# Gathering the first block of tokens before the last two expert tiles are stored

## What is computed

```python
def _moe_ref(x, w_gate, w_noise, noise, w1, w2):
    ...
    for e in range(E):                      # 8 experts
        for k in range(2):                  # a token's two best
            mask = top2[:, k] == e
            h = np.maximum(x[mask] @ w1[e], 0.0)
            out[mask] += top2_w[mask, k, None] * (h @ w2[e])
    return out

def _moe2_ref(x, w_in, w_out):              # x: 1152 x 512, w_in: 512 x 2048
    h = x @ w_in
    g = h * np.cos(h)
    return g @ w_out
```

## Time and profile before

| | before |
|---|---|
| median of 3 runs | 867.7 us (865.75 to 868.94) |
| the profiled execution | 867.97 us, its span 866.2 us |
| PE busy | 845.9 us, 98% of the span |
| DVE, ACT, POOL busy | 493.7, 421.9, 401.3 us |
| granted TensorE clock | 0.998 of full, mean |
| chain that ended last | PE 88%, DVE 5%, ACT 2%, POOL 2% |

### The profile page before, as it was taken

The page is one execution under the profiler, slowest core; times in us unless marked ns, Lnnn a source line. Parts: engine busy times, 40 slices in busy tenths (PEclk is TensorE's granted clock), DMA queues, the critical chain, the costliest instruction groups (busy, mean ns, idle before and its releaser), DMA issues.

```text
span 866.2 us, 15441 instructions
## 1 busy us (share of the span) xinstructions
PE 845.9 (98%) x4894; PEld 751.0 (87%) x4895; DVE 493.7 (57%) x983; ACT 421.9 (49%) x775; POOL 401.3 (46%) x293
## 2 busy tenths in 40 slices
PE   7999999999999989999999999999988999999998
PEld 6899999999999887888888888888877889999897
DVE  6788778887778886323232323232234776575664
ACT  3777777777777763211121112111134565565544
POOL 8554445546787006567959956859022030000000
PEclk9999999999999999999999999999999999999999
DMA  5212111152251017986536636445225020100101
GB/s 133 63 42 79 46 41 41 41 159 63 89 165 49 1 56 236 339 296 222 171 111 219 201 133 194 133 147 181 73 84 183 1 73 1 37 1 0 38 1 37
DMA packets 51377, 90.50 MB, mean 104 GB/s; under 512 B 9360, under 2 KB 18576, under 8 KB 50832
## 3 DMA queue, kind: packets, MB, share of 16 engines
q1 hardware_dynamic: 40688, 66.47, 23.2%
q10 hardware_dynamic: 7296, 12.59, 4.5%
q0 software_dynamic: 3360, 11.01, 4.2%
HBM read 73.00 MB, written 17.06 MB: 104 GB/s over the span
## 4 chain that ended last, share of the span: by engine, by line
PE 88%; DVE 5%; ACT 2%; POOL 2%; issue 1%; DMA 1%; another core or an unknown queue 0%; DVEq 0%; POOLq 0%; ACTq 0%
PE ps L1583 10%; PE ps L1585 10%; PE ps L1584 10%; PE ps L1405 5%; PE ps L1435 4%; PE ps L1451 4%; PE ps L1453 4%; PE ps L1452 4%; PE ps L1436 4%; PE ps L1684 3%; PE ps L1683 3%; PE ps L1682 3%; PE ps L1667 3%; PE ps L1669 3%; PE ps L1668 3%; PE ps L1622 2%
## 5 line engine op out<-in xcount | busy, mean ns | idle before, releaser
L623 POOL TENSOR_TENSOR W<-stage,W 128x2048 fp32r<-128x2048 f32 x32 | 147.2, 4600 | 2.6
L999 DVE TENSOR_REDUCE mx<-ps 128x1 f32<-128x384 f32 x225 | 119.6, 551 | 18.2 <-PE ps L1405 18.2
L1011 DVE TENSOR_TENSOR pl__77<-ps,ph 128x576 fp32r<-128x576 f32 x144 | 108.0, 750 | 33.5 <-ACT ps L775 33.5
L770 ACT ACTIVATE ph<-ps 128x576 fp32r<-128x576 f32 x144 | 93.9, 652 | 53.4 <-PE ps L1436 52.4
L775 ACT ACTIVATE ps<-ps 128x576 f32<-128x576 f32 x144 | 93.5, 649 | 0.0
L844 ACT CAST hh<-ps 128x512 fp32r<-128x512 f32 x50 | 26.9, 590 | 129.4 <-PE ps L1622 125.9
L1451 PE MATMUL ps<-ph,vs 128*65 128x288 f32 x288 | 86.0, 299 | 0.4 <-ACT ot L729 0.4
L1435 PE MATMUL ps<-qat,kt 128*128 128x288 f32 x288 | 83.7, 306 | 1.3 <-ACT qbt L722 0.6
L1453 PE MATMUL ps<-ph,vs 128*65 128x288 f32 x288 | 84.8, 294 | 0.0
L1452 PE MATMUL ps<-pl__77,vs 128*65 128x288 f32 x288 | 84.6, 294 | 0.0
L1583 PE MATMUL ps<-W,hh 128*128 (+1 forms) x200 | 80.0, 400 | 1.8 <-DVE hl L1269 1.8
(11 more groups left out here) (210 smaller groups left out, 1966.6 us busy)
## 6 DMA issues: line engine op xcount, KB each, us to landing
stage<-in_moe_w_dram SPq DMA_DIRECT2D x32, 1024.0 KB
y_slots<-ys ACTq DMA_DIRECT2D x25, 256.0 KB
x_slots<-ring SPq DMA_DIRECT2D x22, 256.0 KB
xs<-x_slots ACTq DMA_DIRECT2D x22, 256.0 KB
kn<-in_k_dram SPq DMA_DIRECT2D x16, 288.0 KB, 3.3
vn<-in_v_dram SPq DMA_DIRECT2D x16, 288.0 KB, 2.9
stage<-in_moe_w_in_dram SPq DMA_DIRECT2D x4, 1024.0 KB
stage<-in_moe_w_out_dram SPq DMA_DIRECT2D x4, 1024.0 KB
```

What stands on the lines that cost most here:

```text
L623: pl.tensor_tensor(W[:, slot, 1, part], stage[:, j % 2, :], W[:, slot, 0, part].bitcast(F32), ALU.subtract).then_inc(w_ready, 1)
L999: ve.tensor_reduce(mx3[:, i:i + 1], ps[:, bank_of(hh, ("m", i)), 0:PIECE], AX_X, ALU.max).then_inc(m_ev, 1)
L1011: ve.tensor_tensor(pl_[:, j % 3, :].rearrange("p (a n) -> p a n", a=2), ps[:, 2 * s_par(hh, j):2 * s_par(hh, j) + 2, 0:HQ], ph[:, j % 3, : ...
```

## The change

The first block of tokens (tiles 0 to 2) is gathered when the first 23 tiles are stored (`LATE = SLOTS_T - 2`). A position at or above 23 x 128 is replaced by 0, and its gate by 0 (`pos_on`, `gate_on`), so a token whose row is in tile 23 or 24 gets nothing for it from the gather. That part comes from two matrices `late_sel` of 128 slots x 384 tokens with a token's gate where its slot is, and 0 elsewhere. DVE makes them from the route table, which SP broadcasts to all partitions as `rtb`. PE multiplies `ys` of tile 23 and of tile 24 with them straight into four PSUM banks (0, 1, 4 and 6, one for each 128 of the 512 numbers), which gives the turned tokens, and adds the turned gathered tokens into the same banks by matmuls with the identity. ACT and DVE then split these banks into `fh` and `fl` at once. The matmuls on old data are gone. SP's handling of the route table moves from behind expert 7's weights to ahead of expert 3's. Blocks 1 and 2 are gathered and turned as before, once all 25 tiles are stored.

```diff
-WARM_Y = 38
-WARM_F = 8
+LATE = SLOTS_T - 2
+X2_BANKS = (0, 1, 4, 6)
...
@@ SP
-            with sp.Fori(3, E) as e:
-                stage_set(WPIECES * e, expert_pieces(e))
             sp.wait_ge(route_done, 1)
...
             sp.dma_start(rt2[:, :, :], route.rearrange("(i p) f -> p i f", p=P)).then_inc(rt_loaded, 16)
+            sp.dma_start(rtb[:, :, :].rearrange("p t f -> p (t f)"),
+                         route[0:BLK, :].rearrange("t f -> (t f)").partition_broadcast(P)).then_inc(rtb_loaded, 16)
+            with sp.Fori(3, E) as e:
+                stage_set(WPIECES * e, expert_pieces(e))
@@ POOL
-            pool.wait_ge(y_stored, 16 * SLOTS_T)
+            pool.wait_ge(y_stored, 16 * LATE)
             for i in range(TT):
+                if i == BLK_T:
+                    pool.wait_ge(y_stored, 16 * SLOTS_T)
@@ ACT
             def tile_steps(t, first=False, left=3, more=None, stored=0):
+                if left == 0:
+                    scale_first(0)
+                    scale_first(1)
                 move_h(t)
                 if not first:
                     store_y(t - 1)
+                if left == 0:
+                    scale_first(2)
...
-            for step in TILE_STEPS:
-                for i, part in step:
-                    (scale_first, high_f)[part](i)
+            for c in range(DC):
+                act.wait_ge(bt_done, c + 1)
+                sc.copy(fh[0][:, c, :], ps[:, X2_BANKS[c], 0:BLK]).then_inc(bh_ev, 1)
@@ DVE
+            def late_tiles():
...
+                dve.wait_ge(rtb_loaded, 16)
+                for k in range(2):
+                    for n in range(2):
+                        last = ve.scalar_tensor_tensor(late_n[:, n, :], rtb[:, :, n], late_slot[:, k:k + 1], rtb[:, :, 2 + n],
+                                                       ALU.is_equal, ALU.mult)
+                    then(last)
+                    then(ve.tensor_tensor(late_sel[:, k, :], late_n[:, 0, :], late_n[:, 1, :], ALU.add))
...
             def tile_steps(t, left=3, first=False):
+                if left == 1:
+                    late_tiles()
                 low_h(t)
+                if left == 0:
+                    add_second(1)
+                    add_second(2)
+                    low_out(0)
+                    low_out(1)
...
+                if left == 1:
+                    add_second(0)
...
+            for c in range(DC):
+                dve.wait_ge(bh_ev, c + 1)
+                ve.tensor_tensor(fl[0][:, c, :], ps[:, X2_BANKS[c], 0:BLK], fh[0][:, c, :].bitcast(F32), ALU.subtract
+                                 ).then_inc(bl_ev, 1)
...
+                if g == 0:
+                    dve.wait_ge(y_stored, 16 * SLOTS_T)
@@ PE
+            def late_rows(k):
+                pe.wait_ge(y_ev, LATE + k + 1)
+                for c in range(DC):
+                    last = pe.matmul(ps[:, X2_BANKS[c], 0:BLK], ys[:, c * P:(c + 1) * P], late_sel[:, k, :],
+                                     start=(k == 0), stop=(k == 1))
+                    if k == 1:
+                        last.then_inc(bt_done, 1)
+            def add_tokens(i):
+                pe.wait_ge(x2_done, i + 1)
+                for c in range(DC):
+                    last = pe.matmul(ps[:, X2_BANKS[c], i * P:(i + 1) * P], yg[:, i, 0, c * P:(c + 1) * P], ident[:, :],
+                                     start=False, stop=False)
+                last.then_inc(ft_done, 1)
             def tile_steps(t, left=3):
                 turn_h(t)
...
+                if left == 0:
+                    late_rows(0)
+                    add_tokens(0)
+                    add_tokens(1)
                 expert_out(t)
+                if left == 0:
+                    add_tokens(2)
+                    late_rows(1)
...
-            for i in range(WARM_Y):
-                pe.matmul(ps[:, 3, :], hh[:, i % FC, :], W[:, 0, 0, 0:BANK], start=True, stop=True)
-            for m in range(BLK_T):
-                turn_tokens(m)
-                for i in range(WARM_F):
-                    pe.matmul(ps[:, 3, :], hh[:, i % FC, :], W[:, 0, 0, 0:BANK], start=True, stop=True)
```

More of the change, by code:

```diff
@@ L388, in build @@
         assert at <= REGION + REGION_BYTES
+        assert at <= XD + 10240
+        rtb, at = place("rtb", XD + 10240, [P, BLK, 4])
+        late_sel, at = place("late_sel", at, [P, 2, BLK])
+        assert at <= REGION + REGION_BYTES
+        late_n, at = place("late_n", REGION + BLK_T * 2 * DM * 4, [P, 2, BLK])
         yg, at = place("yg", REGION, [P, BLK_T, 2, DM])
@@ L861, in high_half, with scale_first @@
                 sc.copy(W[:, 1, 0, at:at + HALF], stage[:, j, part * HALF:(part + 1) * HALF]).then_inc(oh_done, 1)
+            def scale_first(i):
+                act.wait_ge(gather_in[i % BLK_T], 16 * (i // BLK_T + 1))
+                first = yg[:, i % BLK_T, 0, :]
+                gate = gate_on[:, i, 0:1] if i < BLK_T else rt2[:, i, 2:3]
+                sc.activation(first, first, ACT.Copy, scale=gate).then_inc(xa_done, 1)
             def tile_steps(t, first=False, left=3, more=None, stored=0):
+                if left == 0:
+                    scale_first(0)
+                    scale_first(1)
                 move_h(t)
@@ L891, in _ @@
             store_y(SLOTS_T - 1)
[L894 to L898, removed]
             def high_f(i):
@@ L1276, in move_y, with add_second @@
                 ve.tensor_copy(ys[:, :], ps[:, 5, :]).then_inc(y_ev, 1)
+            def add_second(i):
+                dve.wait_ge(xa_done, i + 1)
+                dve.wait_ge(second_in[i % BLK_T], 16 * (i // BLK_T + 1))
+                first = yg[:, i % BLK_T, 0, :]
+                gate = gate_on[:, i, 1:2] if i < BLK_T else rt2[:, i, 3:4]
+                ve.scalar_tensor_tensor(first, yg[:, i % BLK_T, 1, :], gate, first, ALU.mult, ALU.add).then_inc(x2_done, 1)
+            def late_tiles():
+                dve.wait_ge(rt_loaded, 16)
+                then(ve.scalar_tensor_tensor(pos_on[:, :, :], rt2[:, 0:BLK_T, 0:2], float(LATE * P), rt2[:, 0:BLK_T, 0:2],
+                                             ALU.is_lt, ALU.mult))
+                ve.scalar_tensor_tensor(gate_on[:, :, :], rt2[:, 0:BLK_T, 0:2], float(LATE * P), rt2[:, 0:BLK_T, 2:4],
+                                        ALU.is_lt, ALU.mult)
+                ve.tensor_copy(pos2_u[:, BLK_T:TT, :], rt2[:, BLK_T:TT, 0:2])
+                ve.tensor_copy(pos2_u[:, 0:BLK_T, :], pos_on[:, :, :]).then_inc(rt2_done, 1)
+                for k in range(2):
+                    last = ve.tensor_scalar(late_slot[:, k:k + 1], tok[:, 0:1], float((LATE + k) * P), None, ALU.add)
+                then(last)
[4 more added lines that the diff above has]
+                                                       ALU.is_equal, ALU.mult)
+                    then(last)
+                    then(ve.tensor_tensor(late_sel[:, k, :], late_n[:, 0, :], late_n[:, 1, :], ALU.add))
             def tile_steps(t, left=3, first=False):
+                if left == 1:
+                    late_tiles()
                 low_h(t)
+                if left == 0:
[3 more added lines that the diff above has]
+                    low_out(1)
                 if first:
@@ L1308, in _ @@
                 tile_steps(SLOTS_T - 1 - left, left=left)
[L1312 to L1317, removed]
             def low_f(i):
                 blk, m = divmod(i, BLK_T)
-                dve.wait_ge(fh_ev, i + 1)
+                dve.wait_ge(fh_ev, i - BLK_T + 1)
                 ve.tensor_tensor(fl[blk % 2][:, :, m * P:(m + 1) * P],
```

26 lines of the change are left out of this document (13 added, 13 removed).

## The result

| | before | after |
|---|---|---|
| median | 868.2 us (4 runs, 865.75 to 868.94) | 857.12 us (4 runs, 856.61 to 859.45) |
| ratio, 95% interval | | 0.9889 [0.9874, 0.9904] |
| the profiled execution | 867.97 us, span 866.2 | 856.61 us, span 854.9 |
| mean granted TensorE clock | 0.998 | 0.998 |

The changed kernel is 11.1 us faster by the medians and 11.4 by the profiled executions. Forecast were 12.8 and 855.2 us.

What follows compares the result with a forecast made beforehand. PE bounds both stages; between them a chain of waits leaves 19.41 us holding nothing needed but twelve transposes. Last stage starts at 644.5, not 657.33: 867.97 - 12.8 = 855.2 us, range 852 to 859, own range 853.5 to 857.

Steps and rivals of the forecast that it cites:

- The stretch behind is rigid: Last stage to the end: PE busy 204.79 of 208.90 us, so starting it x earlier ends the kernel x earlier.
- Rival C: Last stage: block 0 held by its own chain or block 1's gathers, not PE's start; 864 us, chance 0.06.
- Gathers 20.0 us earlier: POOL: all six gathers wait for 23 stores, not 25; first issue at 621.70, not 641.69.
- Stall for `hl`: PE ahead of tile 23's output, waiting for DVE's low part behind the gate matrices: 0.3 us, bounds 0 and 1.0.
- Plain fp32: PE's `late_rows`: eight instructions of 384 columns at 0.33 us, 2.65 us in all, bounds 1.4 and 2.7.
- 2.93 us ahead of the last tile: PE: `late_rows(0)`, `add_tokens(0)` and `(1)` delay tile 24's output from 632.37 to 635.3, 0.3 us of stall included.
- `add_tokens(2)` hides the copy, the splits are hidden: PE: 0.9 us of `add_tokens(2)` covers tile 24's copy; bank splits covered with 0.2 us to spare.
- rival B: Hand-over: waits for gathers or a late signal before ACT's splits give back 2 to 4 us; 858.2, chance 0.20.
- SP's order costs nothing: SP's early route table: cost 0, up to 2 us of POOL's time covered; expert 3's first piece still released by PE.
- The lock: POOL and DVE: the first gather ends 1.1 us late and moves the other five; ACT's cover holds by 0.7 us.
- The clock: PE without matmuls on old data: the granted clock stays at 1.00 throughout.
- rival D: PE: matmuls on old data kept the clock; slower without them, one short stretch 2 us, at worst 925; chance 0.04.

Runs made afterwards that it cites:

- e3: After with the gate matrices made from 384 numbers side by side in `rtb`, not every fourth (gates then wrong, same work): 855.97 us, one run.
- e4: After with the six larger gate-matrix instructions moved behind `low_h(23)` on DVE: 855.37 us, ratio 0.9858; again 855.08 us, 0.9856.
- e5: After with `ys` and `late_sel` in fp32r, which rounds the late tiles' rows and gates: 853.88 us, one run.
- e2: After with SP's route table and the new broadcast put back behind expert 7's weights: 857.42 us, ratio 0.9874 to before.
- e6: Before with only SP's route table handling moved ahead of expert 3's weights, without the broadcast: 868.68 us, ratio 1.0007.
- after again: The changed kernel unchanged, run a second time on another chip: 857.56 us, ratio 0.9873 to before.
- e1: Before without its 62 matmuls on old data, nothing else changed: 869.41 us, ratio 1.0020.
- e8: Before without the 8 matmuls on old data behind the third turn of tokens, the others kept: 868.25 us, ratio 1.0008.
- e7: After without the gate matrices and both `late_rows`, so the first block lacks tiles 23 and 24: 853.49 us, one run.

## Why the prediction was right, and where it was off

The mechanism, its place and the sign held; 857.12 lies in the range, 1.9 us above the forecast and 0.1 above the forecast's own range of 853.5 to 857. By its steps:

- **The stretch behind is rigid.** Right: 208.6 and 208.8 us, and in all ten profiles without a fallen clock 208.6 to 208.9. Rival C is out. That the gathers' place makes the gain, and not the turn of the tokens straight into four banks, is read from the rows (the earlier trace rows against those above); no run has late gathers with the four banks, so the two are not priced apart.
- **Gathers 20.0 us earlier.** Right: 621.99 for 621.70, 0.28 of which is the start offset. The token data is ready in time.
- **Stall for `hl`, forecast 0.3 us, bounds 0 to 1.0.** This step was mis-sized: 1.31 us marked, 1.59 by the starts of the rows. The price of a `scalar_tensor_tensor` over 384 columns was taken from rows whose operands lie side by side; here both operands are every fourth number of `rtb`: 0.86 us, not 0.55. I had the access pattern in the diff and did not bound it. e3 shows that this is 1.1 us of it; even with `hl` ready when forecast (6.44 us behind the turn, forecast 6.42) PE lost 0.48 by the rows, not 0.3. e4 shows what the whole stall was worth.
- **Plain fp32, forecast 0.33 us an instruction.** Right: eight instructions with 2.68 us to the next group, 0.334 each. The Trainium skill (FP8 and Floating Point Precision, TensorE Precision Notes) says that true fp32 makes four passes; the trace agrees as far as it can: 2.68 us, against the estimate of 2.7 from four passes, and e5's fp32r needs four instructions and 0.80 us for the same product. It shows no single pass.
- **2.93 us ahead of the last tile.** Measured from the turn of tile 24 to the output's first matmul: 631.43 to 636.77, 5.34 us, before 629.56 to 632.37, 2.81: 2.53 us more, where the forecast without its 0.3 had 2.63.
- **`add_tokens(2)` hides the copy, the splits are hidden.** Right: the copy of tile 24 ends at 643.21, 0.06 us ahead of `late_rows(1)`, and the last stage follows with no idle time. The cover is thin: with 1.9 us less in front of it, e5, a wait of 0.73 appears. The late signal of the earlier trace rows, which rival B feared in front of the new splits, did not come: ACT's first copy begins at 644.22, 0.28 us behind the point where the first bank's two instructions are through by their spacing (643.27 + 2 x 0.335).
- **SP's order costs nothing.** Right in the time (e2, e6). The reason given was half right: in after POOL waits for data there and not for PE.
- **The lock.** The first gather was not slowed (0.98 us), the second and fifth were, by 0.3 and 0.2. Both ended 0.82 us behind the DVE instruction that ran when they began: 624.51 behind 623.68, 628.46 behind 627.64. ACT's cover held with 3.1 us, not 0.7. In e4 the first gather takes 1.41 us for the same reason and PE doesn't see it. The Trainium skill (SBUF — State Buffer, SBUF: two separate sides) has the loser blocked for the whole instruction; the two slowed issues agree. The first, begun 0.03 us after a DVE instruction of 0.86 us, does not, here as in e2, e5 and after again, and no run here tells why.
- **The clock.** 1.00 in all of the last stage, rival D did not come. e1 and e8 show that its danger was real: in e1, idle for 9.40 us, PE starts the last stage at half its clock, and in e8 the clock falls one us into it. There it cost 1.6 and 1.1 us, near the 2 us that D gave one short stretch.

So the 1.3 us between 12.8 and 11.5 (the second matmul, 657.61 to 646.13) are 1.3 for the stall (1.59, not 0.3) and 0.3 for the offset with which the profiled execution reached the hand-over. Against them stand 0.1 saved ahead of the last tile and 0.1 from measuring at the second matmul. The median lies 0.5 us above the profiled execution besides. There is some luck in the size: the profiled execution of before had the longer of the two hand-overs of the old order, by 0.7 us; against e6's the change is worth 11.1 us and not 11.8.

## What to carry to other kernels

When all data must be stored before it can be gathered, gather early without the last tiles and add their rows from on chip, by a gate matrix on an engine that would wait anyway. That keeps PE busy with real work, and here the clock held without matmuls on old data. Put what such a correction needs behind whatever PE is waiting for, and read the stride of its operands before you price it: a row of the same operation and width is no price for another access pattern.

## What the runs showed of the hardware that I had not expected

- A `scalar_tensor_tensor` over 384 fp32 columns takes 0.55 to 0.6 us with operands side by side and 0.86 us when both are every fourth number.
- A copy released by the third turn's signal began 1.99 us (before) and 1.24 us (e6) behind the turn with eight matmuls queued behind it, and 0.3 us behind it with none (e8). The second turn, also with eight behind it, had no such delay. In e1, where no turn has anything behind it, the third copy also starts as soon as its turn ends (658.39 + 1.09, and 659.52).
- An indirect gather's issue takes 0.95 us alone; one that begins while DVE runs an instruction on two SBUF tiles mostly ends some 0.82 us behind it. The first one of after is the exception, 0.98 us.
- The last store took 4.15 us, not 2.84, to be seen by POOL when it went beside the staging of the second half of `w_out`; the stretch 643 to 646.7 moved 299 GB/s. In the other versions of the changed kernel it took 3.65 (e2) to 6.16 us (e7). The cause was not tested.
